# Moving the rank products and the placing of the routing within a fused attention, MLP and mixture-of-experts kernel

## What is computed

```python
keep = is_sink | in_window
a = softmax(where(keep, scale * q @ k.T, -1e9))      # attn_out = a @ v
a = x @ w1; b = x @ w2
x = ((a * b) @ w3) @ w_out
logits = x @ w_gate + modality_bias[modality_id]
e_idx = argmax(logits, axis=1)                       # gate_w: its softmax probability
out[mask] = gate_w[mask, None] * (relu(x[mask] @ w1[e]) @ w2[e])
```

## Time and profile before

| | |
|---|---|
| Time, median of 3 runs | 882.04 us (881.56 to 885.13) |
| The profiled execution's own time | 881.52 us |
| Its span, first to last instruction | 879.8 us |
| Busy in the span: PE, DVE, ACT, GpSimd | 864.5, 623.3, 381.6, 178.3 us |
| Mean granted clock of PE | 0.998 |

### The profile page before, as it was taken

The page is one execution under the profiler, slowest core; times in us unless marked ns, Lnnn a source line. Parts: engine busy times, 40 slices in busy tenths (PEclk is TensorE's granted clock), DMA queues, the critical chain, the costliest instruction groups (busy, mean ns, idle before and its releaser), DMA issues.

```text
span 879.8 us, 22177 instructions
## 1 busy us (share of the span) xinstructions
PE 864.5 (98%) x7992; PEld 810.2 (92%) x7992; DVE 623.3 (71%) x1482; ACT 381.6 (43%) x925; POOL 178.3 (20%) x289
## 2 busy tenths in 40 slices
PE   7999999999999999999999999999999999999996
PEld 5788999999999999999999999999999999999994
DVE  6766876875876875875876873348877777777774
ACT  4556534333333343343442442243455555555555
POOL 2352212222212222212222221101100000000001
PEclk9999999999999999999999999999999999999999
DMA  8735623123123123033123021152561113511111
GB/s 232 211 121 161 225 61 97 48 84 103 32 85 109 47 86 108 26 91 104 56 82 92 30 81 61 37 193 61 160 225 48 48 48 108 178 48 48 48 49 37
DMA packets 94296, 82.86 MB, mean 94 GB/s; under 512 B 51070, under 2 KB 74112, under 8 KB 94208
## 3 DMA queue, kind: packets, MB, share of 16 engines
q1 hardware_dynamic: 89728, 68.02, 26.4%
q0 software_dynamic: 4192, 13.66, 4.2%
q10 hardware_dynamic: 288, 0.00, 0.0%
HBM read 56.18 MB, written 25.54 MB: 93 GB/s over the span
## 4 chain that ended last, share of the span: by engine, by line
PE 97%; DMA 1%; ACT 1%; DVE 0%; issue 0%; POOLq 0%; SPq 0%; ACTq 0%
PE acc_a L344 7%; PE acc_b L344 7%; PE acc_a L346 6%; PE acc_b L346 6%; PE acc_a L345 6%; PE acc_b L345 6%; PE misc L340 4%; PE misc L338 4%; PE misc L339 4%; PE s_even L1006 3%; PE acc_a L338 3%; PE acc_b L338 3%; PE acc_b L340 3%; PE acc_b L339 3%; PE attn L339 2%; PE attn L340 2%
## 5 line engine op out<-in xcount | busy, mean ns | idle before, releaser
L866 POOL TENSOR_TENSOR probs<-scores,row_inv 128x256 f32<-128x256 f32 x96 | 67.2, 720 | 278.3 <-DVE row_inv L1975 278.3
L1448 ACT ACTIVATE ew<-raw_e 128x1024 fp32r (+1 forms) x92 | 93.1, 1050 | 12.0 <-issue 10.9
L344 PE MATMUL acc_a<-xT_w,w 128*128 128x384 f32 x256 | 89.4, 349 | 0.0
L344 PE MATMUL acc_b<-xT_w,w 128*128 128x384 f32 x256 | 87.9, 343 | 0.0
L346 PE MATMUL acc_a<-xT_w,w 128*128 128x384 f32 x256 | 86.6, 338 | 0.0
L346 PE MATMUL acc_b<-xT_w,w 128*128 128x384 f32 x256 | 86.5, 338 | 0.0
L345 PE MATMUL acc_a<-xT_w,w 128*128 128x384 f32 x256 | 86.5, 338 | 0.0
L345 PE MATMUL acc_b<-xT_w,w 128*128 128x384 f32 x256 | 86.5, 338 | 0.0
L1474 ACT ACTIVATE scores<-scores,neg_max 128x136 f32<-128x136 f32 x192 | 75.9, 397 | 20.6 <-DVE neg_max L1965 20.6
L1448 ACT ACTIVATE uT_w<-ab 128x384 fp32r<-128x384 f32 x64 | 33.3, 520 | 92.5 <-DVE ab L2027 92.5
L942 POOL DMA_INDIRECT out<-row_out,ids_i x24 | 25.6, 1065 | 222.5 <-DVE row_out L2144 212.1
(11 more groups left out here) (393 smaller groups left out, 2911.2 us busy)
## 6 DMA issues: line engine op xcount, KB each, us to landing
raw_e<-in_moe_w SPq DMA_DIRECT2D x24, 512.0 KB, 7.9
raw<-in_moe_w SPq DMA_DIRECT2D x16, 512.0 KB, 6.2
x_in<-routed SPq DMA_DIRECT2D x100, 64.0 KB, 2.1
v_nat<-in_v SPq DMA_DIRECT2D x24, 256.0 KB, 3.0
x_mid<-x_out SPq DMA_DIRECT2D x24, 256.0 KB, 2.0
x_in<-x_mid SPq DMA_DIRECT2D x24, 256.0 KB, 2.8
q_nat<-in_q SPq DMA_DIRECT2D x80, 64.0 KB, 2.3
k_nat<-in_k SPq DMA_DIRECT2D x80, 64.0 KB, 2.0
```

The lines of the kernel that those rows point to most:

```text
L344: pe.matmul(o, w_hi, x_hi, start=start, stop=False, skip_group_check=True)
L866: pool.tensor_tensor(probs[:, at, side * HALF:(side + 1) * HALF], scores[:, at, side, SINKS:], row_inv[:, at].unsqueeze(2).broadcast_to([P ...
L1448: return act.activation(o, i, ACT.Copy)
```

## The change

Two calls are moved, in rounds 1 to 6. `route_rank(g - 1)` on PE stood behind `mlp_b(g, 0)` and now stands behind `mlp_a(g, 2)`, directly ahead of the turning of ta's probabilities. `route_place(g - 1)` on DVE stood behind the split of part 0 and now stands behind that of part 2. The calls for the last two groups, in round 7 and behind it, stay where they were. Nothing is added or removed.

```diff
@@ tensor
                 mlp_b(g, 0)
                 if g == 0:
                     gate_sum(FOLD - 2)
-                else:
-                    route_rank(g - 1)
                 mlp_a(g, 1)
                 mlp_b(g, 1)
...
                 mlp_a(g, 2)
                 if g == 0:
                     gate_parts(FOLD - 1)
+                else:
+                    route_rank(g - 1)
                 attn_probsT(ta)
                 mlp_b(g, 2)
@@ vector
                 mlp_uT(g, 0)
-                if g > 0:
-                    route_place(g - 1)
                 mlp_u(g, 1)
                 mlp_uT(g, 1)
                 take_probsT(ta, 0)
...
                 turn_qk(tb)
                 mlp_u(g, 2)
                 mlp_uT(g, 2)
+                if g > 0:
+                    route_place(g - 1)
                 if g == 0:
                     gate_weights(FOLD - 1)
                 sum_x(ta)
```

## The result

The changed kernel takes 901.77 us (median; 901.45 to 905.93), beside 882.31 us for the kernel before: a ratio of 1.0227, with a 95% interval of 1.0195 to 1.0258. That is 2.3% slower. The forecast was 1.7% slower, 897.1 us. The direction was right, and the time lies at the upper edge of the range of 891 to 902; by the ratio, 1.0227 times the 882.04 us that the forecast started from, it is 902.1, just past it. The profiled execution took 901.45 us, with a span of 899.8 us against 879.8 before. Two executions, one of e2 (4827.75 us) and one of e4 (1208.49 us, at a mean clock of 0.656), were in a slow state and are left out of every median and ratio here.

The account below looks back on a forecast made before the run. PE was taken to bound the kernel, without a wait in the main loop. Even rounds 5.9 plus odd rounds 9.6 less 0.4 for the rank products gave 15.1 us, so 897.1 us, 1.7% slower, range 891 to 902.

Parts of the forecast that it names:

- Whatever makes PE wait adds its whole length: PE, rounds 1 to 6: PE is issued without a gap, so each wait costs its full length, six times at most.
- Even rounds: Rounds 2, 4, 6: attn_values(ta) waits for the late reading of the ranks, 1.95 us a round, 5.9 us in all.
- The restart: Even rounds: PE's restart after waiting for the ranks, with no row for it, bounded by 0 and 0.3 us.
- Odd rounds: Rounds 1, 3, 5: placing, send, carry_keys, own_v_sinks and take_v_sinks in order delay tb, 3.2 us a round, 9.6 in all.
- the three rounds are alike: Odd rounds: rounds 3 and 5 were taken to repeat round 1 with the same intervals.
- The slack of tb's sink transposes: Odd rounds: 0.48 us, the smallest slack, taken off the 3.67 us delay to leave 3.19 us lost.
- `mlp_uT(g, 2)` became short: DVE, odd rounds: without GpSimd beside it, it was to take 0.56 us instead of 1.46.
- The small waits of PE: Odd rounds, behind the stall of about 2.5 us: small waits on ACT's copy of acc_a and on GpSimd's L866 or L870.
- The rank products: PE, rounds 1 to 6: their new place behind the third a-half saves 0.07 us a round, 0.4 in all, ends 0 and 0.9.
- 3.1 us without work did not lower it. My longest single stall is 2.5: Granted clock: still 2.4 GHz after 3.1 us idle at the kernel's end, so no fall was counted behind stalls.
- by that rule too these stalls would just pass: Granted clock: the skill's advice against idle gaps over about 3 us was taken to let stalls up to 2.5 us pass.
- the clock falls: Rival, 6 in 100: odd stalls bring 1.2 GHz, halves b4 and a5 take twice as long, 4.2 us a round, 909.8 us.

Follow-up runs that it names:

- e2: Changed kernel, but GpSimd issues each round's first send behind the normalising of tb: 891.94 us, ratio 1.0094.
- e4: Changed kernel with the edits of e2 and e3 together: 883.20 us, ratio 1.0004.
- e6: e2 with the reading of the ranks put between mlp_u(g, 2) and mlp_uT(g, 2), so PE waits less: 884.71 us, ratio 1.0037.
- e1: Changed kernel with the rank products put back behind the first b-half, the placing still late: 902.63 us, ratio 1.0226.
- e3: Changed kernel with only the reading of the ranks put ahead of the turning of q and k, the rest of the placing late: 894.51 us, ratio 1.0125.
- e7: Changed kernel with each round's first send directly behind carry_keys(tb) and own_v_sinks, ahead of tb's normalising: 891.97 us, ratio 1.0115.
- e5: Changed kernel with small extra products on PE where it would wait, 32 in even rounds and 44 in odd: 900.12 us, ratio 1.0210.
- e10: e7 with 32 small extra products on PE ahead of the wait for the ranks in even rounds: 891.41 us, ratio 1.0110.
- e8: e7 with the reading of the ranks early, behind take_probsT(ta, 1), as in e3: 882.34 us, ratio 1.0005.
- e9: Kernel before, both calls in their old places, with only the send moved as in e7: 885.37 us, ratio 1.0038.

## Why the prediction was right or wrong

**What bounds the kernel.** "Whatever makes PE wait adds its whole length": e6 bears this out, with 2.4 us of stalls and 2.9 us lost. At stalls of 1.9 us and more it was too little, as below.

**Even rounds.** Right in place and in size. DVE's third part started when it did before, counted from PE's products, and could not use the room that the placing had left; the reading of the ranks stood behind it; PE was idle for 1.92 to 1.94 us and fell back by 2.0 us a round, against 1.95. The restart, for which I had bounds of 0 and 0.3 us, was 0.15 us from the end of the reading (243.77 + 0.17 to 244.09). The sum of x shifted and no second stall came, as worked out.

**Odd rounds.** Right in mechanism and in size: 3.55, 3.18 and 3.17 us against 3.2, and e2 takes them away by one call moved on GpSimd. From `place_i` to the next GpSimd instruction the forecast had 0.96 + 1.1 us. In rounds 3 and 5 it was 0.96 + 1.03, and in round 1 it was 1.14 + 1.21, which explains that round's greater loss; that the three rounds are alike did not hold there. The slack of tb's sink transposes took up about what was worked out for it. `mlp_uT(g, 2)` became short (0.56 us), as forecast. The small waits of PE that were forecast behind the stall don't appear.

**The rank products.** A saving of 0.4 us was about right: their old place gave back the 0.15 us a round that was read from the rows, and the new one cost 0.10, so 0.3 us in all. It is too little for the times: e1 shows that the half of the change made on PE is worth nothing that can be measured.

**The step that failed** is "3.1 us without work did not lower it. My longest single stall is 2.5", and with it "by that rule too these stalls would just pass". The granted clock did fall behind stalls of 1.9 to 2.65 us: in the profiled executions behind 2 of the 6 in the full change and in e1, 2 of 3 in e2, all 3 in e3, 1 of 3 in e7, so 10 of 21. It fell behind none of the three of 0.8 us in e6, and behind none where PE was given work (e5, e10) or had no stall (e4, e8, e9). A row at the kernel's end, where no work followed, was read as proof for places in the middle of dense work, and it isn't one. The row just behind it, in the same trace of before, shows the clock down, while PE was idle still:

```profile
876.00:880.00 4.00, 0.00 (x0) 0.00 (x0) 0.00 (x0) 0.00 (x0) 0.00 (x0) 0.50 0.00 0
```

So that idle stretch did lower the clock, 3.1 us after PE's last matmul. In the twelve traces the clock fell 2.1 (e7) to 5.2 us (e1) after PE's last matmul: one reading of it says little about the next. The advice of the Trainium skill in "TensorE: Matmul & The Clock Gate", section "Why this matters for your kernels", to avoid idle gaps over about 3 us, is too lax for this kernel; the measurement decides. The rival "the clock falls" had the mechanism, and its price was far too high: it let the two halves behind each odd stall run at 1.2 GHz from end to end, 4.2 us a round. It also had a fall only behind the longer, odd stalls, and in the full change one of the two is behind an even one. In the traces a fall cost 1.5 to 1.6 us in an even round (the full change, e1, e2, e7) and 0.75 to 0.9 in an odd one (the full change, e3), so 2.3 us for the whole kernel.

**What was not thought of** is the pause of PE beside a send. The late placing moves the send from a place beside long half products, where no row shows a pause, to one beside tb's short score matmuls. It costs 0.8 us each in rounds 2 and 6.

So both waits were sized to 0.4 us in 15.5, and the 4.9 us that the sum lacked are the clock (2.3), the pauses (1.6), the start-up of that one execution (0.6), the waits (0.4) and the rank products (0.1), less 0.1 elsewhere. The sum had put the first two at nothing.

**What stays open.** Why the clock fell behind some stalls of equal length and not behind others isn't known; e3 and e2 show that it differs by kernel, and executions of one kernel differ too (0.988 to 0.995). The scatter at the kernel's end shows that the time from idleness to a fall is not a fixed one. Why a send's issuing holds PE was not tried. Neither was a kernel that keeps the placing late and has only the pause taken away. The profiled execution of e3, the slowest of its four, lost 1.6 us more behind the rounds, between 671 and 679, for which no cause is known.

## What to carry to other kernels

Where an engine bounds the kernel and never waits, moving small work on another engine gains nothing and may lose, so look for each semaphore that the moved work signals and for each instruction that stands behind its consumers in an in-order list: here one reading of 24 columns and one send in front of an unrelated preparation made both waits. If such work has to move, split off the piece that frees the shared buffer (e3) and move the consumer behind what doesn't depend on it (e2); both together cost nothing that can be measured (e4, e8). And add to a stall of about 2 us on TensorE the chance of a fall of the clock, some 0.8 to 1.6 us each time that it comes, and don't take an idle stretch at the kernel's end for evidence against it.

## What was not expected of the hardware

- The granted clock fell to 1.2 GHz behind 10 of 21 stalls of 1.9 to 2.65 us, and behind none of 0.8 us (e6). With small products that filled the stalls no stretch of e5 or e10 shows a fall, and the mean clock was 0.997 to 0.999 in all nine executions.
- In each of the twelve traces the clock fell after PE's last matmul of the kernel, between 2.1 us (e7) and 5.2 us (e1) later.
- The issue of an indirect DMA on GpSimd (1.03 us busy) was followed 0.8 us after its start by a pause of 0.5 us in PE's short matmuls (32x204); six sends so placed cost 3.4 us (e9), though only the three of the even rounds show such a pause. Beside long matmuls (128x384) no pause is seen.
- In the full change, GpSimd's next instruction started 1.21 us (round 1) or 1.03 us (rounds 3 and 5) behind such an issue, and the issue 1.14 or 0.96 us behind the DVE instruction that it waited for.
